# Three stages of one kernel: a new order for the opening, an earlier start of the last stage's softmax, and weight loads into tiles as they come free

## The reference, cut to what matters

```python
# attention: q, k, v, f_logit (4, 8, 768, 48)
f = 1 / (1 + exp(-f_logit))
state = f[t] * state + outer(k[t], v[t]);  y[t] = q[t] @ state
# x: (3072, 384); w1 (4, 384, 1024), w2 (4, 1024, 384), shares p (3072, 4)
for e in range(4):
    out += p[:, e:e+1] * (maximum(x @ w1[e], 0) @ w2[e])
# x = out; phi (384, 32), v1 (8, 384, 1024), v2 (8, 1024, 384)
logits = x @ phi
d = softmax(logits, axis=0);  slots = d.T @ x          # 32 x 384, four rows per expert
s = per expert: maximum(slots @ v1[e], 0) @ v2[e]      # 32 x 384
out = softmax(logits, axis=1) @ s
```

## Time and profile before

| what | value |
|---|---|
| median of 3 runs | 1057.5 us (1057.32 to 1059.19) |
| the profiled execution's own time | 1060.31 us |
| its span, first to last instruction | 1058.6 us |
| TensorE busy by the page | 1019.7 us (96%) |
| VectorE, ScalarE, GpSimd busy | 358.6, 278.0, 87.5 us |
| chain that ended last, share of TensorE | 93% |
| mean granted TensorE clock | 0.978 of 2.4 GHz |
| moved by DMA | 67.04 MB |

### The profile page before, as it was taken

One profiled execution on the slowest core, in us unless ns is written; L12 is line 12 of the kernel. 1 busy time (PEld: TensorE's weight loads), 2 busy tenths in 40 slices (PEclk: granted clock), 3 DMA queues, 4 the chain that ended last, 5 costly groups with the idle time before them and its releaser, 6 DMA issues.

```text
span 1058.6 us, 17785 instructions
## 1 busy us (share of the span) xinstructions
PE 1019.7 (96%) x6997; PEld 964.5 (91%) x6997; DVE 358.6 (34%) x773; ACT 278.0 (26%) x577; POOL 87.5 (8%) x109
## 2 busy tenths in 40 slices
PE   6799999999999999999999999999999999999895
PEld 5698999999998999999999999999999999999443
DVE  5556556455553222222222222222222222222323
ACT  4433333333321411111123111111322222222322
POOL 2340001000000500000014000000410000000000
PEclk9799999999999999999999999999999999999797
DMA  8732523334313030000002000000030004020785
...
DMA packets 129761, 67.04 MB, mean 63 GB/s; under 512 B 106656, under 2 KB 125088, under 8 KB 129696
## 3 DMA queue, kind: packets, MB, share of 16 engines
...
## 4 chain that ended last, share of the span: by engine, by line
PE 93%; SPq 3%; DVE 2%; issue 1%; ACT 0%; DMA 0%; DVEq 0%; ACTq 0%
PE ph L1275 13%; PE po L1293 13%; PE po L1295 13%; PE ph L1277 13%; PE ph L1276 13%; PE po L1294 13%; PE pair L1225 2%; PE pc L1251 2%; PE pc L1256 2%; PE pc L1194 1%; PE ph L1427 1%; PE po L1442 1%; PE pair L1233 1%; PE pc L1196 1%; PE pair L1207 1%; PE pair L1211 1%
## 5 line engine op out<-in xcount | busy, mean ns | idle before, releaser
L999 DVE SCALAR_TENSOR_TENSOR h_lo<-ph,h_hi 128x384 fp32r<-128x384 f32 x256 | 142.7, 557 | 520.4 <-ACT h_hi L764 519.6
L1275 PE MATMUL ph<-xT,w_hi 128*128 128x384 f32 (+1 forms) x768 | 265.8, 346 | 2.2 <-DVE xT L980 2.2
L764 ACT ACTIVATE h_hi<-ph 128x384 fp32r<-128x384 f32 x256 | 125.9, 492 | 523.8 <-PE ph L1277 523.8
L1293 PE MATMUL po<-w_hi,h_hi 128*128 128x384 f32 x768 | 261.5, 341 | 0.0
L1277 PE MATMUL ph<-xT,w_lo 128*128 128x384 f32 (+1 forms) x768 | 257.7, 336 | 0.0
L1276 PE MATMUL ph<-xT,w_hi 128*128 128x384 f32 (+1 forms) x768 | 257.6, 335 | 0.0
L1295 PE MATMUL po<-w_hi,h_lo 128*128 128x384 f32 x768 | 257.0, 335 | 0.0
L1294 PE MATMUL po<-w_lo,h_hi 128*128 128x384 f32 x768 | 256.8, 334 | 0.0
L1275 PEld LDWEIGHTS ph<-xT,w_hi 128*128 128x128 f32 x768 | 144.9, 189 | 10.7 <-issue 7.9
L1293 PEld LDWEIGHTS po<-w_hi,h_hi 128*128 128x128 f32 x768 | 144.2, 188 | 2.6 <-issue 1.3
L1276 PEld LDWEIGHTS ph<-xT,w_hi 128*128 128x128 f32 x768 | 145.1, 189 | 0.0
(11 more groups left out here) (169 smaller groups left out, 709.3 us busy)
## 6 DMA issues: line engine op xcount, KB each, us to landing
...
```

The source lines that it names most:

```text
L764: a.activation(h_hi[:, f % 2, :], ph[f % 2][:, 0:BLK], ACT.Relu).then_inc(h_hi_done, 1)
L999: d.scalar_tensor_tensor(out=h_lo[:, f % 2, :], in0=ph[f % 2][:, 0:BLK], scalar=0.0, in1=h_hi[:, f % 2, :].bitcast(F32), op0=ALU.max, op1= ...
L1275: t.matmul(bank, wh, xh, start=(kk == 0), stop=False, skip_group_check=True)
L1293: t.matmul(bank, hh, w2_hi[:, f, :], start=(f == 0), stop=False, skip_group_check=True)
```

## The change

In the opening, the first expert's weights come in four loads of two f-tiles each (R0, R2, R4, R6), R0 behind Y1; h and s pieces begin inside `OPENING` (h0.0, h0.1, s0.0) and units 5, 6 and 7 become short; X of half 7 goes ahead of the last three pieces. x and w1 get layouts in which a half of x and an f-tile of w1 are contiguous, so that either can be overwritten when it is done. In the last stage the maxima, exponentials and sums of tiles 0 to 17 are taken during the last block; the six last tiles follow with their own maximum, and the early slots are scaled by the exponential of the difference. The logits of the last half come straight from x. The inverse of the column sum is applied in the relu of the first products. The combine weights are turned as they are, 128x128, high and low; the output is three matmuls of 32 rows per tile, four tiles in four row groups. The fold of L1353 comes one f-tile earlier. Loads of v2(3), v1(4), v2(4), v1(5) go in parts into f-tiles of the last expert's weights while the last block runs.

```diff
 OPENING = (
-    "G0 L0 G1 C0 D0 L1 T0 T1 S0 P0 S1 P1 C1 D1 R0 Y0 Y1 G2 T2 T3 L2 S2 P2 S3 P3 C2 Y2 D2 Y3 G3 "
-    "W0 T4 L3 W1 S4 P4 W2 X0 Y4 C3"
+    "G0 L0 G1 C0 D0 L1 T0 T1 S0 P0 S1 P1 C1 D1 Y0 Y1 R0 T2 T3 G2 S2 P2 S3 P3 L2 Y2 Y3 C2 D2 R2 W0 "
+    "T4 S4 P4 W1 X0 h0.0 G3 Y4 h0.1 W2 s0.0 L3 R4 W3 C3"
 )
 HALVES, UNITS, PER_HALF = 8, 32, 4
 LAG = 5
-SPLITS = {5: (3, 4), 6: (5, 6), 7: (7,)}
-SHORT = (14, 22)
+SPLITS = {5: (4,), 6: (5, 6), 7: (7,)}
+SHORT = (5, 6, 7, 14, 22)
 ...
 for u in range(LAG, UNITS + 1):
-    n = 4 * (u - LAG) - sum(1 for w in SHORT if w < u)
+    n = begun + 4 * (u - LAG) - sum(1 for w in SHORT if w < u)
     if u == UNITS:
-        steps += pieces[n:]
+        last = pieces.index(("h", HALVES - 2, f_tiles - 1))
+        steps += pieces[n:last]
+        steps.append(("X", HALVES - 1, None))
+        steps += pieces[last:]
         break
 ...
 steps.append(pieces[n + 1])
+if u == LAG:
+    steps.append(("R", f_tiles - 2, None))
 if u % PER_HALF == 0:
 ...
-    steps.append(("X", HALVES - 1, None))
 ...
-xT = at("xT", [P, B, 2, KT, S], F32R, r_x)
+X_HALF = 2 * KT * BLK * 4
+xT = at("xT", [P, B, 2, 2, KT, BLK], F32R, r_x)
+w1_hi = at("w1_hi", [P, FT, KT, P], F32R, r_w)
+w1_lo = at("w1_lo", [P, FT, KT, P], F32R, r_w + W1_PART)
 ...
 combine_bank = [po[2], bST]
-ring = [ph[0], ph[1], po[0], po[1], bT, bSY]
+ring = [ph[0], ph[1], po[0], po[1], po[2], bT, bSY, bST]
 ...
+mixture = [("slots", 0), ("inverse", 0), ("first", 0)]
 for x in range(E2):
     if x + 1 < E2:
         mixture.append(("first", x + 1))
     mixture.append(("turn", x))
-    if x < NT // 4:
-        mixture.append(("combine", x))
-    mixture.append(("second", x))
-PE_AT = {name: PE_SLOTT + 1 + i for i, name in enumerate(mixture)}
-PE_PICK = PE_SLOTT + len(mixture) + 1
+    if x:
+        mixture.append(("second", x - 1))
+mixture.append(("second", E2 - 1))
 ...
-    sp.wait_ge(h_filled, step_of(E - 1, B - 1, 1, FT - 1) + 1)
-    sp.dma_start(v1_sb[3][:, 1:KT, :], v1_dram[3, :, 1:KT, :]).then_inc(v1_in[3], 16)
-    load_v2(3)
-    load_v1(4)
-    load_v2(4)
+    sp.wait_ge(h_filled, step_of(E - 1, B - 1, 0, FT - 1) + 1)
+    load_v1(3)
+    def rows_of_v2(e, f0, f1):
+        sp.dma_start(v2_sb[e][:, f0:f1, :], v2_dram[e, :, f0:f1, :]).then_inc(v2_in[e], 16)
+    def part_of_v1(e, kk):
+        sp.dma_start(v1_sb[e][:, kk:kk + 1, :], v1_dram[e, :, kk:kk + 1, :]).then_inc(v1_in[e], 16)
+    for kk, (f0, f1) in enumerate(((0, 3), (3, 6), (6, FT))):
+        sp.wait_ge(h_filled, step_of(E - 1, B - 1, 1, f1 - 1) + 1)
+        rows_of_v2(3, f0, f1)
+        part_of_v1(4, kk)
+        sp.wait_ge(o_step, step_of(E - 1, B - 1, 1, f1 - 1) + 1)
+        rows_of_v2(4, f0, f1)
+        part_of_v1(5, kk)
     sp.wait_ge(pe_c, PE_X2_PART)
-    load_v1(5)
-    sp.wait_ge(pe_c, PE_SLOTS)
     load_v2(5)
+    sp.wait_ge(pe_c, PE_EARLY)
     load_v1(6)
+    sp.wait_ge(pe_c, PE_LATE)
+    load_v2(6)
     sp.wait_ge(pe_c, PE_AT["first", 0])
-    load_v2(6)
+    load_v1(7)
     sp.wait_ge(pe_c, PE_AT["second", 0])
-    load_v1(7)
-    sp.wait_ge(pe_c, PE_AT["first", 3])
 ...
-            act.dma_start(raw1_0[:], w1_dram[0]).then_inc(raw_in, 16)
-            act.dma_start(raw2_0[:], w2_dram[0]).then_inc(raw_in, 16)
+            cols = slice(i * P, (i + 2) * P)
+            act.dma_start(raw1_0[:, :, cols], w1_dram[0, :, :, cols]).then_inc(raw0_in[i // 2], 16)
+            act.dma_start(raw2_0[:, i:i + 2, :], w2_dram[0, :, i:i + 2, :]).then_inc(raw0_in[i // 2], 16)
 ...
+    def early_step(f):
+        if f == 3:
+            act.wait_ge(dve_early, E_DEXP)
+            a.activation(dexp[:, 0:EARLY], dexp[:, 0:EARLY], ACT.Exp).then_inc(act_early, 1)
+        if f == 5:
+            act.wait_ge(dve_early, E_CEXP)
+            a.activation(logit[:, 0:EARLY], logit[:, 0:EARLY], ACT.Exp).then_inc(act_early, 1)
 ...
+    def early_step(f):
+        if f == 0:
+            dve.wait_ge(l_taken, 2 * B - 2)
+            d.tensor_reduce(logit[:, NT, :], logit[:, 0:EARLY].rearrange("p i s -> p s i"), AX.X,
+                            ALU.max).then_inc(dve_early, 1)
+        if f == 1:
+            dve.wait_ge(pe_early, 1)
+            d.tensor_reduce(early_col[:], bT[0:SLOTS, 0:P], AX.X, ALU.max).then_inc(dve_early, 1)
+        if f == 2:
+            dve.wait_ge(pe_early, 2)
+            d.tensor_tensor(dexp[:, 0:EARLY], logit[:, 0:EARLY],
+                            bSY[:, 0:SLOTS].unsqueeze(1).broadcast_to([P, EARLY, SLOTS]),
+                            ALU.subtract).then_inc(dve_early, 1)
 ...
+        if f == 5:
+            dve.wait_ge(act_early, 1)
+            d.tensor_reduce(part_sum[:, 0, :], dexp[:, 0:EARLY].rearrange("p i s -> p s i"), AX.X,
+                            ALU.add).then_inc(dve_early, 1)
+        if f == 7:
+            dve.wait_ge(act_early, 2)
+            d.tensor_reduce(row_sum[:, 0:EARLY], logit[:, 0:EARLY], AX.X, ALU.add).then_inc(row_summed, 1)
+            dve.wait_ge(pe_early, 3)
+            d.tensor_copy(early_sum[:], bT[0:SLOTS, 0:1]).then_inc(dve_early, 1)
 ...
+    def last_logits(s):
+        pe.wait_ge(xt_taken, BT * (2 * B - 1) + s + 1)
+        if s == 0:
+            pe.wait_ge(lt_taken, 2 * B - 1)
+        for kk in range(KT):
+            mm = t.matmul(bST[:, s * SLOTS:(s + 1) * SLOTS], x2T[:, kk, s * P:(s + 1) * P], phi_sb[:, kk, :],
+                          start=(kk == 0), stop=(kk == KT - 1))
+        return mm
 ...
+    assert 4 * SLOTS == P
+    def early_slots_of(i0, i1):
+        for i in range(i0, i1):
+            j = i % 4
+            mm = t.matmul(ph[0][SLOTS * j:SLOTS * (j + 1), 0:DM], dexp[:, i, :],
+                          x2v[:, i, :], start=(i < 4), stop=(i >= EARLY - 4))
+        return mm
+    pe.wait_ge(act_early, 1)
+    pe.wait_ge(x2_copied, 2 * B - 2)
+    pe.wait_ge(h_lo_done, step_of(E - 1, B - 1, 1, FT - 1) + 1)
+    early_slots_of(0, 6)
+    turn_rows(2 * B - 1, 1, 0)
+    pe.wait_ge(dve_early, E_SUM)
+    turn_rows(2 * B - 1, 1, 1)
+    last_logits(0)
+    turn_rows(2 * B - 1, 1, 2)
+    last_logits(1)
+    last_logits(2).then_inc(l_filled, 1)
+    n = step(early_slots_of(6, 10))
+    assert n == PE_X2_PART and 8 * DM * 4 == W1_PART
     pe.wait_ge(dve_c, D_PARTMAX)
     n = step(t.transpose(bT[0:SLOTS, 0:P], part_max[:], ident[:]))
     assert n == PE_MAXT
 ...
+    early_slots_of(10, 12)
+    pe.wait_ge(dve_c, D_COLMAX)
+    n = step(t.matmul(bSY[:, 0:SLOTS], col_max[:, 0:1].broadcast_to([SLOTS, P]), ident[0:SLOTS, 0:SLOTS],
+                      start=True, stop=True))
     assert n == PE_MAXB
+    early_slots_of(12, 14)
+    pe.wait_ge(act_c, A_SHRINK)
+    pe.wait_ge(spread_made, 1)
+    n = step(t.matmul(bT[:, P:P + 1], spread[:], shrink_row[:], start=True, stop=True))
+    assert n == PE_SPREAD
+    n = step(early_slots_of(14, EARLY))
+    assert n == PE_EARLY
+    pe.wait_ge(act_c, A_LATE)
     pe.wait_ge(x2_copied, 2 * B)
+    for i in range(EARLY, NT):
+        j = (i - EARLY) % 4
+        mm = t.matmul(po[0][SLOTS * j:SLOTS * (j + 1), 0:DM], dexp[:, i, :],
+                      x2v[:, i, :], start=(i < EARLY + 4), stop=(i >= NT - 4))
     n = step(mm)
 ...
+    pe.wait_ge(act_early, 2)
+    n = step(turn_combine(0))
+    assert n == PE_COMBINE[0]
+    pe.wait_ge(dve_c, D_PARTSUM)
+    n = step(t.matmul(bT[0:SLOTS, 0:1], part_sum[:, 1, :], ones_f[:, 0:1], start=True, stop=True))
+    assert n == PE_COLSUM
+    pe.wait_ge(act_c, A_CLATE)
+    n = step(turn_combine(1))
+    assert n == PE_COMBINE[1]
 ...
+        pe.wait_ge(dve_c, D_TURN[x])
+        pe.wait_ge(v2_in[x], 16 * (3 if x in (3, 4) else 1))
 ...
+    for i in range(0, NT, 4):
         if i >= len(ring):
-            pe.wait_ge((act_out, dve_out)[i % 2], (i - len(ring)) // 2 + 1)
-        n = step(t.matmul(ring[i % len(ring)][:, 0:DM], cT[:, i * P:(i + 1) * P], s3[:], start=True, stop=True))
-        assert n == PE_OUT + i + 1
+            pe.wait_ge(act_out, (i - len(ring)) // 2 + 2)
+            pe.wait_ge(dve_out, (i - len(ring)) // 2 + 2)
+        cols = slice(i // 4 * P, (i // 4 + 1) * P)
+        for n, (c_part, s_part) in enumerate(((cT_hi, s_hi), (cT_lo, s_hi), (cT_hi, s_lo))):
+            for j in range(4):
+                rows = slice(SLOTS * j, SLOTS * (j + 1))
+                mm = t.matmul(ring[(i + j) % len(ring)][:, 0:DM], c_part[rows, cols], s_part[rows, :],
+                              start=(n == 0), stop=(n == 2))
+                if n == 2:
+                    assert step(mm) == PE_OUT + i + j + 1
```

428 lines of the change are left out of this document (237 added, 191 removed).

## The result

The changed kernel takes **1046.4 us** (median of 4 runs, 1044.75 to 1047.27) against 1057.8 for the kernel before (1057.32 to 1059.19); the ratio is 0.9893, 95% interval 0.9875 to 0.9912. It is faster, by 11.5 us where 19.6 were forecast, and lies 0.4 us above the range. The profiled execution took 1044.75 us, its span is 1043.0.

What follows compares the result with a forecast made beforehand. TensorE is full in the middle, so only the opening, the first stage's end and the last stage can pay. Terms 2.5+3.9-0.7+8.6+1.5+4.3-0.5 = 19.6 us off the median 1057.5 give 1037.9 us, range 1032 to 1046.

Steps and rivals of the forecast that it cites:

- The opening: Start of the kernel: earlier stores let x of half 0 be split sooner; 2.5 us gained, bounds 0 to 8.5.
- T4 at its old place: Opening: the transposes of unit 4 come at 34.3 us, where they were before (34.43).
- the low clock once more: Opening: TensorE too little busy before the first h, so its clock falls again, costing up to 3 us.
- T5 at 48.3: Opening: the transposes of unit 5 come at 48.3 us; before at 46.83, but without three pieces.
- X of half 7: End of the first stage: moved ahead, it removes a wait and low-clock matmuls; 3.9 us gained, bounds 2.3 and 4.
- E to the first product: Last stage, from the last MLP sums matmul: 20.8 us becomes 12.2, 8.6 us saved.
- the work put before E: Last block: three small matmuls added for the early maxima and sums cost 0.7 us, bounds 0.3 and 2.
- First product, mixture: Last stage: first product at full clock saves 1.5 us; hidden hT copies and dropped turns save 4.3 us.
- Output: End of the kernel: stores start later behind the twelve matmuls of a group, 0.5 us lost.
- Asking for them earlier is worth 0 by itself: Mixture: the loads of v were never waited for, so issuing them earlier gains 0 by itself.
- The clock in the last stage: Rival, 25%: TensorE's clock falls again in the last stage, serial matmuls take twice their time, +4.5 us, 1042.4.
- the 1 to 2 us: Last stage: eight more tiling-mode changes would drain TensorE, making the stage 1 to 2 us longer than the sum.

Runs made afterwards that it cites:

- a13: Changed kernel with one step moved: the weight load R2 issued later, right behind the split of half 0's x; 1048.89 us, ratio 0.9922.
- a14: As a13, with the third pair's gate and logarithm where they were before the change and C3 behind the first hidden piece alone; 1046.03 us, ratio 0.9897.
- a12: Changed kernel, opening's second half reordered: gate and logarithm early, C3 ahead of the MLP pieces, R2 behind x's split; same kernel as a8; 1044.17 us, ratio 0.9889.
- a5: Changed kernel with only the third pair's logarithm step moved ahead of h0.1 and the second pair's weights; 1044.41 us, ratio 0.9878.
- a10: Changed kernel with the opening's first half in the order before the change, its second half as in the change; 1045.68 us, ratio 0.9896.
- a8: Same kernel as a12, in an earlier group of runs: changed kernel with only the opening's second half reordered; 1040.93 us, ratio 0.9851.
- a2: Changed kernel with X of half 7 put back behind the last pieces; 1050.85 us, ratio 0.9929.
- a7: Changed kernel with the loads into freed f-tiles held until the whole last block is done; 1052.84 us, ratio 0.9957.
- a6: Changed kernel with the early slot matmuls all together behind the spread, none between turns and maxima; 1048.43 us, ratio 0.9913.

## Why the prediction was right and wrong

**The opening: forecast -2.5, measured +2.1. This is the step that failed**, and in it this sentence of the prediction: "x of half 0 can be split as soon as the mask and states of unit 4 are done, 38.9 instead of 41.35". 38.85 is where the mask starts; mask and states end at 40.6 and `x_low` starts at 41.35 in both kernels. The late stores had never held it alone; VectorE arrived at the same moment. So the earlier landing, right as forecast and the main source of the gain, was worth nothing (a13 took the last of the wait for rows away, and TensorE waited as long). What was left of the new order were its costs: the first piece stands in front of Y4 and C3, which could run meanwhile (waits of 3.2 us against 1.9, a14 against a12), and the logarithm and GpSimd's sums stand behind the second weights (C3's waits of 1.5 us, gone in a5). a10 shows that the second half of the order is enough to lose it all. That the longer idle stretch also makes the low clock likelier fits a8 and a12 but is not shown. The smaller claims held: T4 at its old place, C3's wait of 1.5, the low clock once more. The forecast of T5 at 48.3 was 4.8 us too early. The lower bound of the term, 0, excluded a loss, and should not have: no reason did.

**The base: 4.1 us.** The forecast took differences from one profiled execution and subtracted them from the median. The profiled execution of the kernel before was 2.5 us above the median of its kernel's runs, that of the change 1.6 below. So the traces show 15.6 and the medians 11.5. The mean clock tells which kind it was: 0.978, which only the runs of the kernel before at 1059.9 us and more had; its median runs show 0.981 to 0.983 and its fastest (1054 to 1056) 0.983 to 0.986. So a part of the half-clock time that I counted as recoverable is probably absent from most executions; which part, the mean does not tell. With 4.0 from the terms and 0.3 from the reference's median this makes the 8.5 us of the miss.

**X of half 7**: 4.1 for 3.9, and a2 gives it back (4.1 in the trace, 4.6 in the medians). **E to the first product**: 8.1 for 8.6, while the work put before E cost 1.1 for 0.7. **First product, mixture**: 6.3 for 5.8, with 3.09 us per expert. **Output**: the stores bind (DMA share 0.94 in the last 9 us, when the matmuls are done); -0.4 for +0.5.

**"Asking for them earlier is worth 0 by itself" was wrong.** Held back, the loads cost 6.6 us (a7). The likely reason why the v loads had not been waited for is that the old stage gave them 20.8 us before the first product; a stage of 13 does not. A faster stage and its earlier loads are one edit.

**The clock in the last stage** (a rival at 25%): it held at 1.00 in 12 of the 15 traces that have the fill, the profiled one among them. In a8 and a13 it fell near 992 and 998 for some 7 us, and E to the first product took 15.90 us instead of 13.05; in a10 it fell for half as long, and it took 14.34. a8's stretches, which answer to the earlier trace rows:

```profile
992.00:994.00 2.00, 2.00 (x12) 0.39 (x13) 1.32 (x4) 0.35 (x2) 0.82 (x1) 0.58 0.01 2
994.00:996.00 2.00, 2.00 (x8) 0.69 (x6) 0.52 (x3) 0.23 (x2) 0.00 (x0) 0.50 0.82 186
```

So the rival is real in three traces of 15, and its price is 1.3 to 2.9 us, not 4.5. Without the fill it fell in the one trace taken (a6). The Trainium skill (TensorE: Matmul & The Clock Gate, Part 4) says that transposes don't count as busy in the same way for the clock gate. Here turns and gaps alone lost the clock in a6, and turns with slots between them mostly kept it, which fits but doesn't separate turns from gaps. The Trainium skill (TensorEngine Tiling (Array Packing), Key Properties) says that a change of tiling mode drains TensorE. Of the 1 to 2 us that the prediction estimated from this nothing shows: the stretch came out 0.5 us above the sum, with all else that was uncertain in it.
